# One load for each tile's q and k, a separate buffer for the last tile's squares, later splits of x2T, and another order in step 1

## The reference

```python
def _attn_ref(q, k, v, n_sink, window):          # n_sink 4, window 128
    scores = scale * np.matmul(q, k.transpose(0, 1, 3, 2))
    keep = is_sink | in_window                   # the 4 first keys, or the 128 latest
    scores = np.where(keep, scores, -1000000000.0)
    a = np.exp(scores - np.max(scores, axis=-1, keepdims=True))
    a = a / (np.sum(a, axis=-1, keepdims=True) + 1e-09)
    return np.matmul(a, v)

def _moe_ref(x, w_in, w_out, g_ln):              # x 1536 x 512, w_in 512 x 1024
    h = x @ w_in
    sm = softmax(h)                              # over the 1024 columns, with 1e-09
    solu = h * sm
    ln = (solu - mu) / np.sqrt(var + 1e-06) * g_ln
    return ln @ w_out

def _moe2_ref(x, w_in, w_out):                   # w_in 512 x 2048
    r = np.maximum(x @ w_in, 0.0)
    return (r * r) @ w_out
```

## Time and profile before

| | us |
|---|---|
| median of 3 runs | 504.93 (503.52, 504.93, 505.35) |
| profiled execution | 503.79 |
| its span, first to last instruction | 502.1 |
| busy TensorE | 484.4 (96%) |
| busy VectorE | 287.0 (57%) |
| busy ScalarE | 201.1 (40%) |
| busy GpSimd | 95.5 (19%) |

### The profile page before, as it was taken

One profiled execution on the slowest core, in us unless ns is written; L12 is line 12 of the kernel. 1 busy time (PEld: TensorE's weight loads), 2 busy tenths in 40 slices (PEclk: granted clock), 3 DMA queues, 4 the chain that ended last, 5 costly groups with the idle time before them and its releaser, 6 DMA issues.

```text
span 502.1 us, 7334 instructions
## 1 busy us (share of the span) xinstructions
PE 484.4 (96%) x2644; PEld 393.3 (78%) x2644; DVE 287.0 (57%) x513; ACT 201.1 (40%) x532; POOL 95.5 (19%) x138
## 2 busy tenths in 40 slices
PE   8989989999999999999789999999999999999997
PEld 6667667888778888877678888888888888888885
DVE  4999898888898887865693433332222232232222
ACT  3667546545665655433343322421211232221121
POOL 2555051120022202357970000000000000000000
PEclk9999999999999999999999999999999999999999
DMA  8921343452222211038100000020000002000002
GB/s 247 289 66 44 113 146 80 121 162 62 55 61 75 60 40 35 14 84 290 22 4 0 1 0 1 0 84 0 0 0 0 0 0 85 0 1 0 0 1 84
DMA packets 39717, 29.21 MB, mean 58 GB/s; under 512 B 29256, under 2 KB 29256, under 8 KB 39176
## 3 DMA queue, kind: packets, MB, share of 16 engines
q1 hardware_dynamic: 39384, 28.56, 19.6%
q10 hardware_dynamic: 304, 0.27, 0.2%
HBM read 22.52 MB, written 3.15 MB: 51 GB/s over the span
## 4 chain that ended last, share of the span: by engine, by line
PE 76%; DVE 14%; SPq 5%; ACT 2%; issue 2%; POOL 1%; DMA 0%; DVEq 0%; POOLq 0%; ACTq 0%
PE score_ps L1407 24%; PE h_ps L1419 12%; PE h_ps L1214 9%; PE w_ps L1252 7%; PE wt_ps L1419 6%; PE w_ps L1419 6%; SPq L342 4%; PE o_ps L1184 2%; PE score_ps L1156 2%; PE wt_ps L1164 1%; DVE prob L905 1%; PE wt_ps L1156 1%; DVE bstat L862 1%; SPq L399 1%; DVE u L855 1%
## 5 line engine op out<-in xcount | busy, mean ns | idle before, releaser
L1407 PE MATMUL score_ps<-x2T_hi,w2in_hi 128*128 (+1 forms) x192 | 74.8, 389 | 0.0
L1407 PE MATMUL score_ps<-x2T_hi,w2in_lo 128*128 (+1 forms) x192 | 74.7, 389 | 0.0
L1407 PE MATMUL score_ps<-x2T_lo,w2in_hi 128*128 (+1 forms) x192 | 74.7, 389 | 0.0
L1089 DVE TENSOR_TENSOR sq<-relu 128x512 f32<-128x512 f32 x24 | 18.6, 775 | 83.2 <-ACT relu L775 83.2
L1089 DVE TENSOR_TENSOR e<-e 128x512 f32<-128x512 f32 x24 | 18.5, 770 | 79.6 <-ACT e L775 79.6
L775 ACT ACTIVATE relu<-score_ps 128x512 f32<-128x512 f32 x24 | 14.4, 598 | 100.0 <-PE score_ps L1407 100.0
L775 ACT ACTIVATE e<-score_ps 128x512 f32<-128x512 f32 x24 | 14.4, 599 | 90.4 <-PE score_ps L1407 90.4
L1407 PEld LDWEIGHTS score_ps<-x2T_hi,w2in_lo 128*128 128x128 f32 x192 | 36.1, 188 | 7.5
L1407 PEld LDWEIGHTS score_ps<-x2T_hi,w2in_hi 128*128 128x128 f32 x192 | 36.0, 188 | 7.5
L1407 PEld LDWEIGHTS score_ps<-x2T_lo,w2in_hi 128*128 128x128 f32 x192 | 36.0, 188 | 7.3
L600 ACT ACTIVATE prob<-sm,nbias 128x132 f32<-128x132 f32 (+1 forms) x96 | 37.8, 396 | 0.5
(11 more groups left out here) (177 smaller groups left out, 1094.8 us busy)
## 6 DMA issues: line engine op xcount, KB each, us to landing
w2in<-w_in SPq DMA_DIRECT2D x4, 1024.0 KB, 5.1
w2out<-w_out SPq DMA_DIRECT2D x8, 512.0 KB, 7.4
V<-v SPq DMA_DIRECT2D x12, 256.0 KB, 2.7
x2T<-x SPq DMA_DIRECT2D x192, 16.0 KB, 1.8
k_raw<-kT SPq DMA_DIRECT2D x20, 132.0 KB, 2.8
q_raw<-qT SPq DMA_DIRECT2D x20, 128.0 KB, 2.8
w2in<-w_in SPq DMA_DIRECT2D x4, 512.0 KB, 6.5
w2in<-w_out SPq DMA_DIRECT2D x2, 1024.0 KB, 11.7
```

The costliest lines, as they stand in the source:

```text
L1089: nc.vector.tensor_tensor(sq[f % 2], relu[f % 2], relu[f % 2], ALU.mult).then_inc(sq_ready, 1)
L1407: done = mm(h2_ps[f % 2], ws[:, c, fs], xs[:, c, bass.ts(blk, BLK)], start=(c == 0 and i == 0), stop=(c == MC - 1 and i == 2))
```

## The change

Five edits, all in the order or the shape of transfers and instructions; the arithmetic stays.

1. Each pair of half loads of q and k becomes one transfer over 128 partitions. Its DRAM side is rearranged so that the half is the first dimension, then the 64 rows, then the heads of a half, then the positions. All waits for these loads count 16 rather than 32. The load of q of tile 1 is issued by ACT, right after that of tile 0, rather than by SP.
2. The squares of tile 11 are written to `y[3]`, a buffer that is used first at the end of stage B's first block. They no longer wait for tile 10's moves, and stand ahead of `split_w2out(0)` in VectorE's order.
3. `round_x2T` and `split_x2T` of blocks 1 and 2 move from f = 2 and 4 to f = 7 and 11.
4. POOL waits for the layer norm of tile 2 ahead of `build_v_sink(1)`.
5. In `second_step`, VectorE does `split_q(4)` ahead of `square_x2(0)` and `normalize_p(3, 1)` ahead of `hidden_max`; TensorE does the scores of tile 3's last two pairs and `transpose_ln(1)` each one group of `hidden` earlier.

```diff
+X2T_AT = (7, 11)
...
+        def squares_of(t):
+            return y[3] if t == NT - 1 else x2[:, :]
...
+        def by_halves(x):
+            return x.rearrange("d (a c) q -> a d c q", a=2)
+
+        def load_q01(queue, n):
+            queue.dma_start(q01[:, n, :, :], by_halves(qT[n])).then_inc(q01_loaded[n], 16)
...
-                for half in range(2):
-                    rows, heads = half_heads(half)
-                    sp.dma_start(q_raw[rows, :, :], qT[n, :, heads, :]).then_inc(q_loaded, 16)
+                sp.dma_start(q_raw[:, :, :], by_halves(qT[n])).then_inc(q_loaded, 16)
...
-                for half in range(2):
-                    rows, heads = half_heads(half)
-                    sp.dma_start(k_raw[rows, :, :], kT[n, :, heads, :]).then_inc(k_loaded, 16)
+                sp.dma_start(k_raw[:, :, :], by_halves(kT[n])).then_inc(k_loaded, 16)
...
-                for half in range(2):
-                    rows, heads = half_heads(half)
-                    sp.dma_start(k01[rows, n, :, :], kT[n, :, heads, :]).then_inc(k01_loaded[n], 16)
+                sp.dma_start(k01[:, n, :, :], by_halves(kT[n])).then_inc(k01_loaded[n], 16)
...
-            for half in range(2):
-                load_q01(sp, 1, half)
...
-            for half in range(2):
-                load_q01(act, 0, half)
+            for n in range(2):
+                load_q01(act, n)
...
                 if t == 2:
+                    pool.wait_ge(ln_ready, 2 * t + 2)
                     build_v_sink(1)
...
-                if f in (2, 4):
-                    round_x2T(f // 2)
+                if f in X2T_AT:
+                    round_x2T(X2T_AT.index(f) + 1)
...
-                if t:
+                if 0 < t < NT - 1:
                     dve.wait_ge(x2T_moved[(t - 1) // TB], (t - 1) % TB * MOVES + MOVES)
-                nc.vector.transpose(x2[:, :], x2_ps[:, :]).then_inc(x2_squared, 1)
+                nc.vector.transpose(squares_of(t), x2_ps[:, :]).then_inc(x2_squared, 1)
...
                 row_max(3, 0)
+                split_q(4)
                 square_x2(0)
...
                 split_k(4)
-                split_q(4)
+                normalize_p(3, 1)
                 hidden_max(2, 0)
                 hidden_max(2, 1)
                 hidden_max_all(2)
-                normalize_p(3, 1)
...
             chain(0, 0)
+            square_x2(NT - 1)
             split_w2out(0)
-            square_x2(NT - 1)
...
-                hidden(2, 16, 20)
                 score(3, 2)
                 score(3, 3)
+                hidden(2, 16, 20)
+                transpose_ln(1)
                 hidden(2, 20, 24)
-                transpose_ln(1)
```

More of the change, by code:

```diff
@@ L301, in attention_moe_program @@
         block = ctx.enter_context(nc.Block())
+        def squares_of(t):
+            return y[3] if t == NT - 1 else x2[:, :]
         def raw_keys(n):
             return k01[:, 1, :, :] if n == 1 else k_raw[:, :, :]
-        def half_heads(half):
-            return slice(half * D, (half + 1) * D), slice(half * PAIRS, (half + 1) * PAIRS)
-        def load_q01(queue, n, half):
-            rows, heads = half_heads(half)
-            queue.dma_start(q01[rows, n, :, :], qT[n, :, heads, :]).then_inc(q01_loaded[n], 16)
+        def by_halves(x):
+            return x.rearrange("d (a c) q -> a d c q", a=2)
+        def load_q01(queue, n):
+            queue.dma_start(q01[:, n, :, :], by_halves(qT[n])).then_inc(q01_loaded[n], 16)
         @block.sync
@@ L338, in move_x2 @@
                 sp.wait_ge(x2_squared, t + 1)
-                squares = x2[:, :].rearrange("p (c r b) -> p c r b", r=QUADS, b=SQ)
+                squares = squares_of(t).rearrange("p (c r b) -> p c r b", r=QUADS, b=SQ)
                 for i in range(QUADS):
@@ L500, in round_k @@
             def round_k(n):
-                pool.wait_ge(k_loaded, 32 * (n - 1))
+                pool.wait_ge(k_loaded, 16 * (n - 1))
                 pool.wait_ge(k_split, n - 1)
@@ L505, in round_q @@
             def round_q(n):
-                pool.wait_ge(q_loaded, 32 * (n - 1))
+                pool.wait_ge(q_loaded, 16 * (n - 1))
                 nc.gpsimd.tensor_copy(QH[n % 2][:, :, :], q_raw[:, :, :]).then_inc(q_hi, 1)
@@ L581, in round_k @@
             def round_k(n):
-                act.wait_ge(k_loaded, 32 * (n - 1))
+                act.wait_ge(k_loaded, 16 * (n - 1))
                 act.wait_ge(k_split, n - 1)
@@ L587, in round_q @@
             def round_q(n):
-                act.wait_ge(q_loaded, 32 * (n - 1))
+                act.wait_ge(q_loaded, 16 * (n - 1))
                 if since(n, 4):
@@ L721, in round_k1 @@
             def round_k1():
-                act.wait_ge(k01_loaded[1], 32)
+                act.wait_ge(k01_loaded[1], 16)
                 nc.scalar.activation(KH[:, :, KEYS_SINKS[1]], raw_keys(1), ACT.Copy).then_inc(k_hi, 1)
@@ L1110, in _ @@
                 split_w2out(f)
-                if f in (2, 4):
-                    split_x2T(f // 2)
+                if f in X2T_AT:
+                    split_x2T(X2T_AT.index(f) + 1)
                 chain(f + 1, f + 1)
@@ L1130, in score @@
                 if n < 2 and p == 0:
-                    pe.wait_ge(q01_loaded[n], 32)
-                    pe.wait_ge(k01_loaded[n], 32)
+                    pe.wait_ge(q01_loaded[n], 16)
+                    pe.wait_ge(k01_loaded[n], 16)
                 if n >= 2 and p == 0:
```

## The result

The changed kernel takes 539.77 us (median of 4 runs, 537.78 to 540.24); the kernel before takes 504.86 us on the same chip (median of 4, 503.52 to 505.35). The ratio is 1.0688, with a 95% interval of 1.0654 to 1.0722: 34.9 us slower. The forecast was 529, with a range of 511 to 540; the result lies 0.2 us inside its upper end. The profiled execution of the changed kernel took 540.24 us, its span is 538.5.

What follows compares the result with a forecast made beforehand. TensorE was taken as the bound, busy 484.4 of 502.1 us. Profiled 503.79 + 27.7 (part 1) - 2.0 (part 2) - 1.5 (part 3) = 528.0, given as 529 on the median's scale; own range 519 to 537, wider range 511 to 540.

Steps and rivals of the forecast that it cites:

- The two engines: Part 1's q and k loads: a leading dimension of 2 confines each load to two of the 16 DMA engines.
- v_sink_raw's missing landing: DMA issue list: v_sink_raw's load, leading with 24 copies, lacked a landing; taken as a sign that the leading count matters.
- The price of a load: Each q load: 2.6 us fixed plus 5.2 of data on two engines, landing 7.8 us after its issue.
- q(5): Step 1: q(5) lands at 76.0 instead of 71.22, making the projection 3.8 us later.
- The steps t = 4 to 8: ACT rounds q(t+3) ahead of xT in each step; late q loads cost 6.9 us together.
- The argument that a stall moves TensorE but not the next issue: After t = 4: the next issue follows moves made before the stall, so it isn't shifted; q is 0.7 us late.
- The opening: Start through k(3): first score at 14.0 instead of 5.87, further late loads behind it; 17.0 us in sum.
- Rival B: Part 1's load spreads over all 16 engines whatever its leading count; 500.4 us on the median's scale, chance 0.16.
- Rival C: Two engines, but steps from step 1 on absorb late loads; only the opening's 17.0 is paid, 517 us, chance 0.12.
- Rival D: V's share on the two engines, or x2's moves, also late: 2 to 3 us more in six steps, 545, chance 0.04.

Runs made afterwards that it cites:

- the sweep of the leading count: Changed kernel with the one load of q and k leading with 128, 8, 4 or 2 on the DRAM side: 498.0, 501.9, 515.5, 539.8 us.
- the halves: Changed kernel with each load of q and k in two halves again, all else kept: 499.54 us, ratio 0.9879 to the kernel before.
- a lead of 8: Changed kernel with the host's layout in 8 groups of 16 rows, a spare row behind each: 501.86 us, ratio 0.9922 to the kernel before.
- part 3 alone: Kernel before with only x2T's blocks 1 and 2 rounded and split at f = 7 and 11: 504.05 us, ratio 0.9959.

## Why the prediction was right, and where its size was off

**The two engines: right.** Rate, landing, the sweep of the leading count and the halves all say so. The step that took v_sink_raw's missing landing as a sign of it held, though the sign does not give the count: with a lead of 8 the rows of q and k have no landing either. The rule of the Trainium skill that the prediction set beside it ("DMA: Bandwidth & Descriptors", section "Rules for kernel authors") agrees with the 50 GB/s; its line against two transfers to partition halves agrees too, once the one transfer leads with 128 rows: 498.0 against 499.5 us.

**The price of a load: right.** 7.8 us to landing were forecast; q(5) to q(11) took 7.6 to 8.9, q(5) itself 8.8.

**The steps t = 4 to 8: right in the idle time.** Forecast 3.1, 0.7, 1.4, 0 and 1.7 us, 6.9 together; TensorE's waits were 4.21, 0.28, 0.73, 0.50 and 1.36. The 0.28 stands in the trace with halves too, so the late loads added 4.21, 0, 0.73, 0.50 and 1.36, 6.8 together: the sum is nearer than its terms, which is partly luck. The argument that a stall moves TensorE but not the next issue shows in the second of them: against the halves TensorE fell back by 7.9 us from tile 3's squares to tile 4's, the issue of q(8) by only 1.9 more than that of q(7), and q(8) came in time. q(5) cost a wait of 6.08 (0.62 with halves) rather than 3.8 more.

**The opening: near in sum, by luck.** 17.0 us of waiting were forecast, and alone it costs 18.3 by the medians. But in its trace, 19.3 us longer than the halves', TensorE's idle time grew by only 13.9; the other 5.4 are longer products, which the sum did not have. The first score is 16.73 rather than 14.0. Tile 1's q on ACT's queue shared the engines, where the sum had it behind: by 16.7 us ACT's queue had moved 0.36 MB, 0.10 more than q of tile 0, at 50 GB/s an estimated 2 us of the 2.7. And SP's issues stood still, which the sum had at their usual time. Neither was tested alone.

**What the sum left out.** All terms of part 1 together were 27.7 us of waiting; TensorE's idle time grew by 27.4 from the halves to the changed kernel. That they agree so well is luck in part: the forecast had the opening too long (17.0 for 13.9) and the steps a little short (10.7 for 11.5 alone), and 2.0 come only with both. The forecast priced a wait at its own length. The traces show TensorE's products at the lower level of the clock for some 3 to 9 us behind waits of 2.3 to 6.1 us, though not behind the 3.53 in the profile of before: 14.0 us of longer products in all. That is the term that was missing, and with it the result lies above the forecast's own range, 519 to 537: 14.0, less the 2.6 that parts 2 to 5 gained above their 3.5, is the 11 us between 529 and 540.

**Parts 3, 4 and 5: right** (1.5 forecast, 2.1 measured; 1.0 forecast with loads in time, 1.2 measured). **Part 2** was mis-sized in part for the same reason as part 1: 2.0 forecast, 5.7 measured alone (5.2 by the medians). The wait that it removes is 4.1 us in the trace of part 3 alone rather than 3.5, a slow stretch stands behind it, and 0.8 of part 3's wait goes with it. The four do not add up, 9.0 alone (7.7 by the medians) and 6.1 together: that 0.8 is counted twice, and the rest is open.

Rival B's time, 500.4, is that of the kernel with halves, 499.5. Rival C, steps that absorb the late load, holds for t = 5, which waits no longer than with halves, and not for t = 4 (4.21). Rival D's 545 is 5 us too long: V did land later, after 7.6 us rather than 2.7, but no wait of TensorE in the trace is put down to it.

## What to carry to other kernels

Read a load's access pattern from the DRAM side, and put the many rows first: the same 256 KB in one transfer took 2.9 us with 128 rows in front and 7.6 to 8.9 with 2. Allow for a stall of TensorE costing more than its length: read the cadence of the products behind it in the trace, and look at the clock of several executions, not just of the profiled one. And when several edits come together, time them apart: three good ones, 6 us, were hidden here under one that cost 40.

## What the runs showed of the hardware that was not expected

Two issues on SP's queue took 11.87 and 8.03 us while two engines worked off the loads ahead of them; with 128 rows in front the same two took 0.49 and 0.50. So loads that do not lead with 2 were issued late too. Why an issue waits there, no trace shows.

Behind waits of 2.33, 2.98, 4.1, 4.21, 6.04 and 6.08 us TensorE's products started 0.43 us apart rather than 0.23, for some 9, 3, 3, 8, 5 and 6 us; behind the 3.53 of the kernel before they did not. So the length of a wait alone did not tell what it cost. With a lead of 8, where no wait is over 1.7 us, the clock stayed at 1.000.
